# Stage one of a fused recurrent-attention and two-stage feed-forward kernel, cut into seven token steps of two widths instead of eight of one

## The reference

```python
for t in range(S):                                  # S = 768, for each of 4 x 8 heads
    cur = np.einsum('bhd,bhe->bhde', u[None] * kt, vt)
    y[:, :, t] = np.einsum('bhd,bhde->bhe', rt, state + cur)
    state = w[None, :, :, None] * state + np.einsum('bhd,bhe->bhde', kt, vt)
x = y.transpose(0, 2, 1, 3).reshape(3072, 384)
h = ((x @ w1) * (x @ w2)) @ w3                      # w1, w2: 384 x 1024, w3: 1024 x 1024
y2 = h @ w_out                                      # 1024 x 384
h2 = y2 @ w_in                                      # 384 x 2048
out = (h2 * np.cos(h2)) @ w_out2                    # 2048 x 384
```

## Time and profile before

| | us |
|---|---|
| time, median of 3 runs | 795.07 (794.87 to 795.11) |
| the profiled execution | 795.09 |
| its span, first to last instruction | 793.5 |
| TensorE busy | 786.7 |
| VectorE busy | 433.6 |
| ScalarE busy | 380.2 |
| GpSimd busy | 348.2 |

### The profile page before, as it was taken

One profiled execution on the slowest core, in us unless ns is written; L12 is line 12 of the kernel. 1 busy time (PEld: TensorE's weight loads), 2 busy tenths in 40 slices (PEclk: granted clock), 3 DMA queues, 4 the chain that ended last, 5 costly groups with the idle time before them and its releaser, 6 DMA issues.

```text
span 793.5 us, 16222 instructions
## 1 busy us (share of the span) xinstructions
PE 786.7 (99%) x6716; PEld 704.9 (89%) x6716; DVE 433.6 (55%) x650; ACT 380.2 (48%) x663; POOL 348.2 (44%) x287
## 2 busy tenths in 40 slices
PE   8999999999999999999999999999999999999998
PEld 5899999999999999999988888888888888888886
DVE  7998554354444544423379555545555554554553
ACT  4544222232222222223467666656665665665664
POOL 2646647464656556412224444334333432432432
PEclk9999999999999999999999999999999999999999
DMA  8874334242424234031221010001001001001001
GB/s 328 272 243 143 108 89 143 78 123 60 136 69 153 78 96 137 22 100 42 81 85 54 1 40 1 1 0 40 1 0 40 1 0 41 1 0 37 5 0 40
DMA packets 47596, 57.35 MB, mean 72 GB/s; under 512 B 21793, under 2 KB 34210, under 8 KB 47522
## 3 DMA queue, kind: packets, MB, share of 16 engines
q1 hardware_dynamic: 34898, 45.83, 17.8%
q10 hardware_dynamic: 12624, 10.49, 4.3%
HBM read 46.86 MB, written 9.44 MB: 71 GB/s over the span
## 4 chain that ended last, share of the span: by engine, by line
PE 99%; DVE 0%; ACT 0%; issue 0%
PE p_h L1149 25%; PE p_acc L1149 13%; PE p_b L1149 13%; PE p_a L1149 13%; PE p_out L1367 8%; PE p_out L1364 8%; PE p_out L1363 8%; PE p_s L1173 2%; PE p_y L1185 2%; PE p_y L1189 1%; PE p_acc L1297 1%; PE p_kv L1177 1%; PE p_acc L1286 1%; PE p_acc L1283 1%; PE p_acc L1289 1%; PE p_b L1304 0%
## 5 line engine op out<-in xcount | busy, mean ns | idle before, releaser
L617 POOL TENSOR_TENSOR g_l<-g,g_h 128x512 fp32r<-128x512 f32 x96 | 149.8, 1561 | 241.0 <-ACT g_h L801 241.0
L1098 DVE TENSOR_TENSOR g<-angle,p_h 128x512 f32<-128x512 f32 x96 | 65.8, 685 | 109.1 <-ACT angle L810 109.1
L481 POOL TENSOR_TENSOR g_l<-g,g_h 128x384 fp32r<-128x384 f32 x64 | 72.9, 1139 | 117.5 <-ACT g_h L651 117.5
L1149 PE MATMUL p_h<-y_h,wi_h 128*128 128x512 f32 x288 | 112.1, 389 | 0.0
L1149 PE MATMUL p_h<-y_l,wi_h 128*128 128x512 f32 x288 | 112.1, 389 | 0.0
L1364 PE MATMUL p_out<-g_h,wq_h 128*128 128x512 f32 x288 | 112.0, 389 | 0.0
L1363 PE MATMUL p_out<-g_h,wq_l 128*128 128x512 f32 x288 | 112.0, 389 | 0.0
L1149 PE MATMUL p_h<-y_h,wi_l 128*128 128x512 f32 x288 | 112.0, 389 | 0.0
L801 ACT CAST g_h<-g 128x512 fp32r<-128x512 f32 x96 | 59.7, 621 | 67.0 <-PE p_out L1367 42.3
L651 ACT CAST g_h<-g 128x384 fp32r<-128x384 f32 x64 | 32.9, 513 | 115.6 <-DVE g L951 115.6
L806 ACT ACTIVATE angle<-angle 128x512 f32<-128x512 f32 x96 | 60.6, 631 | 49.7 <-DVE angle L1108 49.7
(11 more groups left out here) (118 smaller groups left out, 1669.1 us busy)
## 6 DMA issues: line engine op xcount, KB each, us to landing
krT_raw<-in_kr_dims SPq DMA_DIRECT2D x24, 512.0 KB, 4.2
kr_raw<-in_kr_tokens SPq DMA_DIRECT2D x24, 384.0 KB, 5.0
v_raw<-in_v_tokens SPq DMA_DIRECT2D x24, 192.0 KB, 5.1
x_raw<-y_transposed SPq DMA_DIRECT2D x24, 192.0 KB, 2.6
out<-out_sb SPq DMA_DIRECT2D x17, 256.0 KB, 2.1
stage_b<-in_moe_w_in SPq DMA_DIRECT2D x8, 384.0 KB, 3.1
stage_b<-in_moe_w_out SPq DMA_DIRECT2D x8, 384.0 KB, 2.9
y_transposed<-yT ACTq DMA_DIRECT2D x24, 96.0 KB, 2.6
```

The costliest lines, as they stand in the source:

```text
L481: nc.gpsimd.tensor_tensor(g1_l[:, n % 2, :], g1[:, n % 2, :], g1_h[:, n % 2, :].bitcast(F32), ALU.subtract).then_inc(s_gl, 1)
L617: nc.gpsimd.tensor_tensor(g2_l[:, par, :], g2[:, par, :], g2_h[:, par, :].bitcast(F32), ALU.subtract).then_inc(s_g2l, 1)
L1098: nc.vector.tensor_tensor(g2[:, n % 2, :], angle[:, n % 2, :], p_h[n % 4][:, :], ALU.mult).then_inc(s_g2, 1)
L1149: ins = mm(dst, lhs(x), rhs(y), start=first and q == 0 and p == 0, stop=last and q == len(tiles) - 1 and p == 2)
```

## The change

Stage one is cut into seven steps, of 3, 3, 4, 3, 4, 3 and 4 chunks, that is of 384 or 512 tokens: 56 slots instead of 64. All tiles of a step are as wide as its tokens. The bursts stand in slots 0, 2, 4 and so on up to 40, whatever the step. The splitting of a chunk's x stands three slots behind its burst, or later where the tile that it goes into is still read, at the latest in the last slot but one in front of its use. a is copied into g1, and the gate works in place in g1; copy_a now also waits for the low part that last read this half of g1. To make room, the mask later is kept once and read for all heads by a broadcast; the third slot of stage_b moves into y2's neighbourhood, and tiles of stage two lie elsewhere. In the prologue VectorE's w34_low(1) stands three operations further ahead.

```diff
-X_SLOTS = (3, 5, 6)
+STEPS = (3, 3, 4, 3, 4, 3, 4)
...
-    NSTEP = 2 * NB
+    NSTEP = len(STEPS)
+    FIRST_CHUNK = [sum(STEPS[:j]) for j in range(NSTEP + 1)]
+    WIDTH = [chunks * P for chunks in STEPS]
+    WIDE = max(WIDTH)
...
-    later = sb("later", [P, H, SUB], F32, att)
+    later = sb("later", [P, SUB], F32, att)
...
-    x_raw = sb("x_raw", [P, KT, HT], F32, pa)
+    x_raw = sb("x_raw", [P, KT, HC * P], F32, pa)
...
-    x_h[1] = sb("x_h1", [P, KT, HT], F32R, pa)
-    x_l[1] = sb("x_l1", [P, KT, HT], F32R, pa)
-    a_sb = sb("a_sb", [P, 2, HT], F32, pa)
+    x_h[1] = sb("x_h1", [P, KT, WIDE], F32R, pa)
+    x_l[1] = sb("x_l1", [P, KT, WIDE], F32R, pa)
...
-    B_SLOTS = [stage_b[:, i, :] for i in range(3)]
+    B_SLOTS = [stage_b[:, 0, :], stage_b[:, 1, :], stage_b2[:, :]]
...
-    for j in range(NSTEP - 1):
-        for i in range(HC):
-            n, slot = HC * (j + 1) + i, NF * j + 2 * i
-            bursts[slot] = (n + 1 if n + 1 < NCH else None, n)
-            if n + 2 < NCH:
-                k_at[slot], raw_at[slot + 1], scaled_at[slot + 1], z_at[slot + 2] = n + 2, n + 2, n + 2, n + 2
+    step_of = [j for j in range(NSTEP) for _ in range(STEPS[j])]
+    for n in range(HC, NCH):
+        slot = 2 * (n - HC)
+        bursts[slot] = (n + 1 if n + 1 < NCH else None, n)
+        if n + 2 < NCH:
+            k_at[slot], raw_at[slot + 1], scaled_at[slot + 1], z_at[slot + 2] = n + 2, n + 2, n + 2, n + 2
+        last_used = NF * (step_of[n] - 1) - 1
+        x_at.setdefault(min(max(slot + 3, last_used), last_used + NF - 1), []).append(n)
...
+            if i == 2:
+                sp.wait_ge(s_stl, PIECES_A)
...
-        def copy_a(j, f):
-            act.wait_ge(s_a, NF * j + f + 1)
-            nc.scalar.copy(a_sb[:, f % 2, :], p_a[:, 0:HT]).then_inc(s_acp, 1)
...
+        def copy_a(n):
+            act.wait_ge(s_a, n + 1)
+            if n >= 2:
+                act.wait_ge(s_gl, n - 1)
+            cols = slice(0, WIDTH[n // NF])
+            nc.scalar.copy(g1[:, n % 2, cols], p_a[:, cols]).then_inc(s_acp, 1)
...
-            nc.vector.copy_predicated(scores[:, n % 2, :, :], later[:, :, :].bitcast(I32),
+            nc.vector.copy_predicated(scores[:, n % 2, :, :], later[:, :].bitcast(I32).unsqueeze(1).broadcast_to([P, H, SUB]),
...
+        def gate(n):
+            dve.wait_ge(s_b, n + 1)
+            dve.wait_ge(s_acp, n + 1)
+            cols = slice(0, WIDTH[n // NF])
+            nc.vector.tensor_tensor(g1[:, n % 2, cols], g1[:, n % 2, cols], p_b[:, cols], ALU.mult).then_inc(s_g, 1)
...
         first_states()
+        w34_low(1)
         scale_k_dims(1)
         first_scores()
         scale_r_dims(1)
-        w34_low(1)
         sum_kur(1)
...
-                if f in X_SLOTS and not last:
-                    x_low(j + 1, (j + 1) % 2, X_SLOTS.index(f))
+                for n in x_at.get(slot, ()):
+                    x_low(n)
...
-                ins = nc.vector.tensor_copy(y2[:, t, bass.ds(j * HT, HT)], p_acc[t][:, 0:HT])
+                ins = nc.vector.tensor_copy(y2[:, t, bass.ds(FIRST_CHUNK[j] * P, WIDTH[j])], p_acc[t][:, 0:WIDTH[j]])
...
+        def part_a(bank, wh, wl, n):
+            j, f = divmod(n, NF)
+            cols, width = slice(f * P, (f + 1) * P), WIDTH[j]
+            return split_product(bank[:, 0:width], lambda t: wh[:, t, cols], lambda t: wl[:, t, cols],
+                                 lambda t: x_h[j % 2][:, t, 0:width], lambda t: x_l[j % 2][:, t, 0:width],
                                  [(t, t) for t in range(KT)])
...
-                        pe.wait_ge(s_xl, HC * (j + 2))
...
+                        pe.wait_ge(s_xl, FIRST_CHUNK[j + 2])

```

More of the change, by code:

```diff
@@ L59, in build @@
     HC = CH // 2
-    HT = HC * P
     NCH = NB * CH
@@ L631, in half_masks @@
                 nc.scalar.copy(ident_sub[rows, :], ident[rows, rows]).then_inc(s_halves, 1)
-                nc.scalar.copy(later[rows, :, :], later_all[rows, rows].unsqueeze(1).broadcast_to([SUB, H, SUB])
-                               ).then_inc(s_halves, 1)
+                nc.scalar.copy(later[rows, :], later_all[rows, rows]).then_inc(s_halves, 1)
         def copy_y(n):
@@ L750, in _ @@
         w34_high(7)
-        copy_a(0, 0)
+        copy_a(0)
         piece(6)
-        high(0, 0)
+        high(0)
         piece(7)
@@ L767, in step @@
                 if more:
-                    copy_a(j, f + 1)
+                    copy_a(slot + 1)
                 if last:
@@ L775, in step @@
                 if more:
-                    high(j, f + 1)
+                    high(slot + 1)
                 if bursts.get(slot, (None, None))[1] is not None:
@@ L946, in take_sums, with x_low @@
                 new_state(n, 1)
[L948 to L956, removed]
+        def gate(n):
+            dve.wait_ge(s_b, n + 1)
+            dve.wait_ge(s_acp, n + 1)
+            cols = slice(0, WIDTH[n // NF])
+            nc.vector.tensor_tensor(g1[:, n % 2, cols], g1[:, n % 2, cols], p_b[:, cols], ALU.mult).then_inc(s_g, 1)
+        def x_low(n):
+            j, raw = step_of[n], slice(n % HC * P, (n % HC + 1) * P)
+            cols = slice((n - FIRST_CHUNK[j]) * P, (n - FIRST_CHUNK[j] + 1) * P)
+            dve.wait_ge(s_xh, n + 1)
+            nc.vector.tensor_tensor(x_l[j % 2][:, :, cols], x_raw[:, :, raw], x_h[j % 2][:, :, cols].bitcast(F32),
                                     ALU.subtract).then_inc(s_xl, 1)
@@ L1047, in _ @@
         w34_low(7)
-        gate(0, 0)
+        gate(0)
         piece(6)
@@ L1076, in step @@
                 if not (last and f == NF - 1):
-                    gate(j, f + 1)
+                    gate(slot + 1)
                 if bursts.get(slot, (None, None))[0] is not None:
@@ L1221, in burst, with up_a, up_b, down @@
                             ins.then_inc(s_x[1 - sub], 1)
[L1223 to L1226, removed]
+        def part_a(bank, wh, wl, n):
[3 more added lines that the diff above has]
+                                 lambda t: x_h[j % 2][:, t, 0:width], lambda t: x_l[j % 2][:, t, 0:width],
                                  [(t, t) for t in range(KT)])
-        def up_a(n, par, f):
-            if not (isinstance(n, int) and n == 0):
+        def up_a(n):
+            if n:
                 pe.wait_ge(s_acp, n)
-            part_a(p_a, w1_h, w1_l, par, f).then_inc(s_a, 1)
-        def up_b(n, par, f):
-            if not (isinstance(n, int) and n == 0):
+            part_a(p_a, w1_h, w1_l, n).then_inc(s_a, 1)
+        def up_b(n):
+            if n:
                 pe.wait_ge(s_g, n)
-            part_a(p_b, w2_h, w2_l, par, f).then_inc(s_b, 1)
-        def down(n, f, j):
+            part_a(p_b, w2_h, w2_l, n).then_inc(s_b, 1)
+        def down(n):
+            j, f = divmod(n, NF)
+            width = WIDTH[j]
             pe.wait_ge(s_gl, n + 1)
@@ L1264, in step @@
                 n = NF * j + f
[L1265 to L1267 removed]
+                if not (last and f == NF - 1):
                     if f == NF - 1:
[L1269 to L1275 removed]
+                        pe.wait_ge(s_xl, FIRST_CHUNK[j + 2])
+                    if n + 1 in (2, 4, 6):
+                        pe.wait_ge(s_stl, NWO + n + 2)
+                    up_a(n + 1)
+                    if n + 1 in (2, 4, 6):
+                        pe.wait_ge(s_stl, NWO + n + 3)
+                    up_b(n + 1)
                 if n in bursts:
@@ L1279, in step @@
                     hidden(0, 0, f - (NF - 2))
-                down(n, f, j)
+                down(n)
         def w34_highs(ft, t):
```

82 lines of the change are left out of this document (40 added, 42 removed).

## The result

The changed kernel takes **799.42 us**, the median of 5 runs (798.24 to 801.15); the kernel before, timed beside it, 795.11. The ratio is 1.0056, with a 95% interval of 1.0044 to 1.0067. The forecast of 791.4 us (790.5 to 793.2) is 8 us off and on the wrong side.

What follows compares the result with a forecast made beforehand. TensorE, busy 99% of the span, was taken as the bound: -2.9 us from fewer, wider matmuls and -0.8 from w34's low part, all else 0, took 795.07 to 791.4 us, range 790.5 to 793.2.

Steps and rivals of the forecast that it cites:

- What bounds the kernel: Whole kernel: TensorE, busy 99% of the span, sets the end; an edit counts only through its work or waits.
- Fewer, wider matmuls: Stage one: 1728 matmuls of 384 tokens become 864 of 384 and 648 of 512, saving 2.9 us.
- The bursts and the ring: Stage one: 21 bursts of 2.22 us stay; GpSimd and VectorE finish each denser round within 11.58 us, costing 0 us.
- Gate in place, mask, copies of p_acc: Stage one and the change to stage two: in-place gate, broadcast mask and wider copies delay TensorE nowhere, 0 us.
- w34's low part: Prologue: moving it earlier ends TensorE's wait at tile 3; VectorE then limits, so 0.8 of 1.46 us is gained.
- The rivals: Early gain lost 0.15, or whole 0.07; width gives little 0.03; TensorE waits in stage one 0.10; slower 0.03.
- the one that ends slower (the ring): Stage one: GpSimd and VectorE rounds outgrow their period in 384-token slots; 797.5 us at 2.6 us stretch a round; chance 0.03.

Runs made afterwards that it cites:

- run 6: The changed kernel with 192 B unused ahead of wi_h and 64 B more in over_att, so wi agrees with the rest at 160 modulo 256: 792.72 us, 0.9964.
- run 10: The changed kernel with wi brought to agree with the other tiles, measured once more as a yardstick: 792.50 us, 0.9959 of the kernel before.
- run 1: The changed kernel with over_att 16 floats longer, moving every tile behind wi_h and wi_l by 64 bytes: 792.72 us, 0.9966 of the kernel before.
- run 12: The kernel before with only w34_low(1) moved forward in the prologue: 794.52 us, 0.9989 of the kernel before.

## Where the prediction failed, step by step

**What bounds the kernel: right.** TensorE is busy for 99% of the span in both, and what moved the time was the sum of its matmuls' distances. In runs 6 and 10 its busy time is the 784.0 us that the prediction named; in the changed kernel it is 791.0.

**Fewer, wider matmuls: the mechanism right, the size 2.3 us instead of 2.9.** Up a, up b and down took 303.97 us in the kernel before and 301.71 in run 1, where nothing stands in the way. 27 wide matmuls in a row do take 6.12 us, as taken over from stage two. What the sum left out is what a disturbance costs: without the pauses around the bursts the wide ones average 227.5 ns, not 226.7, which is 0.8 x 648 = 0.5 us. The chain of the changed kernel, where wide steps give way to narrow ones:

```profile
205.20 2.08 PE p_acc L1163 x9
207.29 1.58 PE p_a L1163 x9
```

2.08 us instead of 2.04. In run 1, where all offsets agree, the distances of such a product are 229, 233, 236, 224, 231, 236, 228, 233, 231 ns, and the next wide product is back at 226 or 227; the same row of nine stands in every wide product that follows narrow ones, eight times in stage one, and a shorter one (231, 236, 228, 232, 231) behind each burst in a wide slot. A narrow product behind a wide one loses less, some 0.03 us. Behind a burst in a narrow slot a single matmul shows 176 instead of 173. This price stood in the trace of the kernel before, at the end of stage one, where hidden (512 columns) stands between products of 384:

```profile
393.37 1.56 PE p_b L1149 x9
394.93 2.08 PE p_h L1149 x9
397.01 1.58 PE p_acc L1149 x9
```

The prediction took its 2.04 us from a product further on the earlier trace rows, where the width had long been the same, and didn't read these rows.

**The bursts and the ring: right.** 42.15 us in both, scores 11.58 us apart. The cost that wasn't foreseen is the wait without a releaser behind the new burst in slot 6, 0 to 1.4 us. That the ring needs only 9.4 us stays untested: the prediction added the idle time of two engines to get it, and no run made the ring longer.

**Gate in place, mask, copies of p_acc: right.** TensorE's list of waits has none for g_l, g or y2, and there is no gap at the change to stage two.

**w34's low part: the path right, the size in agreement, -0.8 us against medians of 0.74 and 0.91.** The waits for rT_sc show that VectorE is the limit behind it. The size is not shown closely (0.1 to 1.7 us in run 12), so that it fits so well is in part luck.

**The step that failed: the sum left out a term, the layout of stage two's tiles.** The prediction says nothing of it: the new places of stage two's tiles were in the diff and were never gone through as a part of the change, and stage two itself was read only for the price of a 512-token matmul. That price, 226.7 ns, was used as a property of the matmul. It is one of the matmul and of where its operands lie, and the change moved them: +7.0 us. With it the forecast would have been 795.07 - 2.3 - 0.8 + 7.0 = 799.0 against 799.42 measured. No row of the kernel before showed the price of a disagreement, since everything in it agreed modulo 256; what could have been seen is that a thing held there that no longer held after, and, from 2.08 beside 2.04 us, that the distance of these matmuls isn't fixed by their width. The rivals, too, were all about waits in stage one and the prologue; the one that ends slower (the ring) had nothing to do with what happened, and the 0.03 for slower was that of one mechanism, not of those not thought of.

**The version that beats both.** The changed kernel with 16 floats more in over_att, or with wi moved: 792.5 us in run 10, 792.7 in runs 1 and 6, against 795.0 to 795.3 for the kernel before. Against the forecast of 791.4 us 1.1 are missing: 0.5 in the wide matmuls, 0.1 in narrow products behind wide ones, and 0.5 for which the runs show two candidates and no proof, the wait in slot 6 (0.27 in run 10's profile) and the first loads.

## What to carry to other kernels

Where TensorE sets the end, a change of layout is a part of the change like any other: write down each tile's byte offset before and after, modulo 256, for all tiles that TensorE reads in turn, and keep them equal; unused space of 16 floats in one tile did it here (run 1). Compare the distance between matmul starts (or the page's mean for a group) of the stages that the change does not touch, first of all: 389 against 396 ns told where the 7 us were. Read the price of a matmul also where its length changes. And a term that depends on the first loads is sized by medians of many runs, not by two traces.

## What the runs showed of the hardware

- Back-to-back float32r matmuls (128 x 128 weights, 512 columns) start 226.7 ns apart when all the tiles that they read, weights and moving ones, lie at the same byte offset modulo 256 in the partition and the length has been the same for a while, and 224 to 241 ns when some offsets differ, 229 to 234 on average over hidden's nine. The offset itself doesn't matter among those tried (224, 32 and 160 are alike).
- The loss isn't larger for a larger difference: 66, 20, 90 and 73 ns in eighteen matmuls for the rest at +32, +64, +128 and +192 B against wi.
- It isn't confined to the matmuls whose own tiles disagree: with only project's moving tiles moved, hidden lost 46 ns in nine and project 21, and with only hidden's, project lost 46 and hidden 21 in most slots. And distances of the same sizes (229, 233, 236, 224, 231, ...) appear for nine matmuls after a mere change of width from 384 to 512, all offsets agreeing, in the kernel before as well, and then die out. So it looks like a state that a step in offset or length sets off and that settles if it is left alone; in stage two of the changed kernel a new step comes every nine matmuls. What that state is stays open. The page shows that weights are loaded beside running matmuls (PEld 85 to 89% busy), so that two streams are read at once; that these two meet in some part of the memory would fit, and no run here looked at it directly.
- The Trainium skill ("SBUF — State Buffer", Operand start alignment) asks only that an operand start at a multiple of its element size, and says that this is about legality, not speed. All layouts here fulfil it, and they lie up to 8.7 us apart.
- 384-token products in stage one, whose tiles were always moved together, kept their 173 ns in every layout. What a disagreement would cost them no run shows.
- TensorE can lose 0.3 to 1.4 us inside a product without waiting for any engine or load, behind a run of four bursts of 128 short matmuls each; it does so in some executions only. The cause is open.
